# An unused strip of 192 bytes per partition, so that all large on-chip tiles begin at the same byte modulo 512

## The reference, cut to what matters

```python
scores  = scale * x @ state.T         # per batch (8) and head (8); x 512 x 64, state 32 x 64
a       = softmax(scores);   xread = a @ state
scores2 = scale * state @ x.T
a2      = softmax(scores2);  sread = a2 @ x
x = concat(xread, sread) as rows of 512          # 8 x (512 + 32) rows
h = relu(x @ w_in);  x = (h * h) @ w_out         # first block, 512 -> 2048 -> 512
out = (((x @ w1) * (x @ w2)) @ w3) @ w_out2      # second block, 512 -> 1024 -> 1024 -> 512
```

## The kernel before, in words

| stage | matmuls of 128 x 128 weights | weight from | moving from | columns |
|---|---|---|---|---|
| start, w3 x w_out2 (`multiply_w3`, L590) | 16 x 12 | v | E | 512 |
| first block, h (`h_chunk`, L617), 8 tiles | 16 x 6 a tile | G (GA, GB) | aT | 512 |
| first block, y (`y_chunk`, L625), 8 tiles | 16 x 12 a tile | X | v | 512 |
| attention scores beside it (L541 to L545) | 12 a tile | bd | x | 512 |
| attention, sread (L557 to L562) | 24 a tile | a2T | x | 256 |
| first block of the 256 state rows, h and y | 16 x 12 each | E or G; X | aT; v | 256 |
| second block, a and b (`ab_chunk`, L708), 8 tiles | 8 x 24 a tile | X | E | 512 |
| second block, out (`out_chunk`, L718), 8 tiles | 8 x 12 a tile | v | G | 512 |
| second block of the 256 state rows, a and b | 8 x 24 | X | E | 256 |
| the same, out | 8 x 6 | v | G | 512 |

## Time and profile before

### The profile page before, as it was taken

How to read it: one execution, slowest core, us unless ns; L and a number is a source line. 1 busy time by engine, 2 the same in 40 slices (tenths; PEclk the granted TensorE clock), 3 DMA queues, 4 the chain that set the end, 5 groups by cost and what they waited for, 6 DMA issues and landing times.

```text
span 1312.9 us, 15958 instructions
## 1 busy us (share of the span) xinstructions
PE 1287.8 (98%) x5977; PEld 1051.4 (80%) x5977; DVE 593.4 (45%) x974; ACT 487.0 (37%) x897; POOL 19.4 (1%) x35
## 2 busy tenths in 40 slices
PE   8979999999999999999999999999999999999996
PEld 5657888888888888888889888888888888888886
DVE  6666867565666757565546422212222222222121
ACT  6565554544544545444435321112121212111121
POOL 1000000000000000000000000000000000000000
PEclk9998999999999999999999999999999999999999
DMA  8986431121222121211214221101000100000000
GB/s 293 354 294 211 136 130 53 62 87 49 93 67 80 64 96 49 85 62 44 96 65 153 89 64 49 33 32 33 32 32 32 26 38 12 36 0 32 0 33 16
DMA packets 49815, 105.49 MB, mean 80 GB/s; under 512 B 4072, under 2 KB 5096, under 8 KB 48744
## 3 DMA queue, kind: packets, MB, share of 16 engines
q1 hardware_dynamic: 45464, 84.43, 19.4%
q0 software_dynamic: 4304, 20.45, 4.1%
HBM read 68.16 MB, written 36.70 MB: 80 GB/s over the span
## 4 chain that ended last, share of the span: by engine, by line
PE 95%; DMA 3%; DVE 1%; ACT 0%; issue 0%; SPq 0%; DVEq 0%; ACTq 0%; POOLq 0%
PE ps_y L527 47%; PE ps_h L527 30%; PE ps_t L527 17%; DMA g_scratch<-g_extra 1%; DMA wp_scratch<-stage 1%; DMA g_scratch<-stage 1%; PE ps_t L586 1%; PE ps_h L586 0%; PE ps_t L551 0%; DMA raw<-in_moe_w_in 0%; DVE v_lo L1001 0%; DVE t L1001 0%; ACT v_hi L798 0%; DVE stage L1112 0%; DVE stage L1090 0%
## 5 line engine op out<-in xcount | busy, mean ns | idle before, releaser
L1001 DVE TENSOR_TENSOR t<-t,ps_t 128x512 f32<-128x512 f32 (+1 forms) x72 | 47.4, 659 | 387.3 <-ACT t L798 387.3
L527 PE MATMUL ps_y<-v_hi,X_hi 128*128 128x512 f32 (+1 forms) x576 | 219.7, 381 | 2.1 <-DVE stage L1090 2.1
L527 PE MATMUL ps_y<-v_lo,X_hi 128*128 128x512 f32 (+1 forms) x576 | 219.2, 381 | 0.0
L527 PE MATMUL ps_y<-v_hi,X_lo 128*128 128x512 f32 (+1 forms) x576 | 219.2, 381 | 0.0
L1001 DVE TENSOR_TENSOR v_lo<-t,v_hi 128x512 fp32r<-128x512 f32 (+1 forms) x216 | 143.1, 663 | 155.2 <-ACT v_hi L798 155.2
L798 ACT CAST v_hi<-t 128x512 fp32r<-128x512 f32 (+1 forms) x216 | 128.8, 597 | 192.4 <-DVE t L1001 192.4
L798 ACT COPY t<-ps_h 128x512 f32<-128x512 f32 (+2 forms) x78 | 46.7, 598 | 398.0 <-PE ps_t L527 394.4
L884 ACT ACTIVATE t<-ps_h 128x512 f32<-128x512 f32 (+1 forms) x144 | 82.7, 574 | 166.9 <-PE ps_h L527 166.7
L1001 DVE TENSOR_TENSOR t<-t 128x512 f32<-128x512 f32 (+1 forms) x144 | 95.0, 659 | 103.4 <-ACT t L884 103.1
L527 PEld LDWEIGHTS ps_y<-v_hi,X_hi 128*128 128x128 f32 x576 | 109.0, 189 | 23.7 <-issue 2.5
L527 PEld LDWEIGHTS ps_y<-v_lo,X_hi 128*128 128x128 f32 x576 | 108.7, 189 | 21.0
(11 more groups left out here) (157 smaller groups left out, 1879.5 us busy)
## 6 DMA issues: line engine op xcount, KB each, us to landing
raw<-g_scratch SPq DMA_DIRECT2D x64, 256.0 KB
raw<-in_moe_w_in SPq DMA_DIRECT2D x32, 256.0 KB
raw<-in_x_T SPq DMA_DIRECT2D x32, 256.0 KB
raw<-in_x_tok SPq DMA_DIRECT2D x32, 256.0 KB
y_scratch<-stage POOLq DMA_DIRECT2D x8, 1024.0 KB, 5.7
raw<-y_scratch SPq DMA_DIRECT2D x32, 256.0 KB
out<-stage POOLq DMA_DIRECT2D x8, 1024.0 KB, 4.2
g_scratch<-g_extra SPq DMA_DIRECT2D x14, 512.0 KB, 6.5
```

The source lines that it names most:

```text
L527: mm = nc.tensor.matmul(dst, w, m, start=first and n == 0, stop=last and n == 2)
L1001: return nc.vector.tensor_tensor(dst, a, b, op)
```

## The change

One tile of 48 float32 (192 bytes in each partition) that nothing reads or writes is placed behind `d2`. All tiles behind it move up by 192 bytes: x_hi and E_hi begin at 160896, GA at 193664, st_hi and GB at 210048, each 128 modulo 512. No instruction is added, removed or moved; only addresses in x, s1, aT, a2T, e2, E, G, st and g_extra change.

```diff
@@ -96,6 +96,7 @@
         d1 = sb("d1", [P, HG * TB])
         m2 = sb("m2", [P, HG])
         d2 = sb("d2", [P, HG])
+        sb("line", [P, 48])
         with ExitStack() as attention:
             x_hi = sb("x_hi", [P, PAIRS, S], F32R, attention)
             with ExitStack() as softmax1:
```

## The result

The changed kernel takes 1292.69 us (median of 4 runs, 1292.21 to 1293.25) against 1314.01 for the kernel before (4 runs, 1313.48 to 1314.56): a ratio of 0.9838, 95% interval 0.9821 to 0.9855, 21.3 us. In a second set the ratio was 0.9836 (0.9822 to 0.9850), with 1292.2 us for the changed kernel (median of 4 executions, 1291.43 to 1293.46, without two disturbed ones of 1588 and 4504 us). 1291.1 us was forecast.

What follows compares the result with a forecast made beforehand. The prediction took TensorE, busy 98% of the span, as the bound: matmul count times the distance between starts. Gains of 15.4, 8.3, 0.5 and 0.2 less losses of 1.3, 0.3 and 0.2 made 22.6 us: 1291.1 us, range 1286 to 1303.

Steps and rivals of the forecast that it cites:

- Part 1: Second block, 8 tiles of 288 matmuls: 233.3 to 226.7 ns each, a gain of 15.4 us.
- part 5: 256-column products of the state rows: equal starts are slower, losing 1.3 us in a and b, 0.3 in h, 0.2 in out.
- Part 2: First block, h and y chunks: 4.15 to 4.08 us each, 9.0 us gained less 0.7 for new starts, net 8.3.
- part 3: Attention scores: six matmuls go from 1.39 to 1.36 us, a gain of 0.5 us.
- part 6: VectorE and ScalarE writes of x, E and G at new addresses: hidden by TensorE; half a microsecond either way, nothing taken.
- Part 4: The w3 product, 8 matmuls in 1.84 us: at best 0.6 us gained, 0.2 us taken.
- Addresses do nothing: Rival for the whole kernel: placement is indifferent or the strip does not arrive; time as now, 1313.7 us; chance 0.06.
- Equal starts are the slow case: Rival: 512-column matmuls with equal starts take 240 ns in long streams; 39.7 us slower, 1353.4 us; chance 0.04.
- The second block stays in its rate: Rival: second block keeps 233.3 ns even with equal starts; only 7.2 us gained, 1306.5 us; chance 0.10.
- Thrown out all the time: Rival: 512-column streams settle but keep being unsettled, averaging 229.2 ns; 10.7 us gained, 1303.0 us; chance 0.12.

Runs made afterwards that it cites:

- G alone: Against the kernel before, 192 unused bytes between E and GA: G starts at 128 modulo 512, x and E stay at 448; 1301.53 us.
- E alone: Against the kernel before, x and E moved to start at 128 modulo 512 by the 192-byte strip, G kept at 448 by 320 more; 1303.16 us.

## Why the prediction was right, step by step

**The bound and the count.** TensorE is still at 98%, with the same 5977 matmuls; no wait of another engine grew into the place of what went, but for one (below). The sum was 22.6 us; the profiled executions differ by 1314.48 - 1292.21 = 22.3, the medians by 21.3. That 22.3 is so near is in part luck: it holds 0.9 us at the start that are not the change's, about what the tiles of the first block came short (both below).

**Part 1, second block: right.** The rate of nine settled matmuls in a y chunk was the rate of 2304 in a row. Less the losses of the state rows, 13.9 us were forecast and 14.1 came. The state rows lost what part 5 priced: a and b 1.44 for 1.36, out 1.39 for 1.37, h 1.44 for 1.42.

**Part 2, first block: the mechanism right, the term too large.** With part 3 and the loss of h, 8.5 us were forecast and 7.0 came. Two terms were mis-sized. The gain per chunk, "4.15 less 4.08", was taken from rounded rows as 0.07 us (the trace's nanoseconds give 4.147 less 4.080), and the cost of each new start as 0.03. After the change y reads 2.75 behind sread as assumed, but 2.77 behind the first transposes of a tile and 2.75 to 2.76 behind the second, up to 0.05 over the settled 2.72. A tile gained 72.86 - 71.87 = 0.99 us, not the 1.1 of the sum. The scores went from 1.39 to 1.36, as part 3 has it. And in tile 0 a wait took the place of gained time, which no row of before had been asked for:

```profile
168.29 1.36 PE ps_h L528 x6
169.65 0.12 issue
169.77 3.10 PE ps_t L528 x24
```

The sread of batch 1 took 2.87 us before and takes 0.35 more now, the gap ahead of it included. The timeline of VectorE and of the weight loads after:

```profile
168.82 0.69 DVE L1002 TENSOR_TENSOR a2T_lo<-ps_t,a2T_hi 128x512 fp32r<-128x512 f32 x1
...
169.74 0.19 PEld L528 LDWEIGHTS ps_t<-x_hi,a2T_hi 128*128 128x128 f32 x1 [0.51 <-issue]
```

VectorE's last split of a2T ends at 169.51, when the h ahead of sread has 0.14 us left, and the first weight load starts at 169.74. Before, the split ended at 170.82 and sread started at 171.56, 0.74 us later. So in tile 0, with the weights still to be split beside the attention, VectorE gained 1.3 us on the clock and TensorE 1.8, and the cover of 0.74 us was used up. The profile names no releaser for the gap; it calls it issue. That it is the split is read from two more traces: in the second execution of the changed kernel and with G alone, sread starts 0.26 and 0.25 us behind the split's end, as here, and with E alone, where TensorE comes later, 0.74 us behind it and without a gap. The prediction named VectorE's idle time for part 6 only, and from other tiles.

The border between the first two rows of the table is not firm. The second execution of the changed kernel has the same two rows as follows:

```profile
L528 PE MATMUL ps_h<-aT_hi,GA x288: 283/389/501, 100.5 to 706.7; 128*128 128x512 f32 x128, 128*128 128x256 f32 x16
L528 PE MATMUL ps_h<-E_hi,X_hi x288: 277/389/396, 719.8 to 1274.5; 128*128 128x512 f32 x128, 128*128 128x256 f32 x16
```

Its first block starts 2.2 us earlier and its second only 0.8, for TensorE waits longer in tile 0 for VectorE and ScalarE (3.2 us for `stage` and 1.4 for `g_extra`, against 2.2 and 0.5). So the two rows are best taken together: 8.2 us gained, 9.0 in that execution, and 8.7 forecast. The tile distance of 0.99 us for 1.1 is the firmer sign that the term was too large.

**Part 4 and the start.** The chains before and after, at the first load and at a w3 chunk:

```profile
1.40 5.63 DMA raw<-in_moe_w_in
...
22.99 2.96 PE ps_y L527 x12
```

```profile
1.40 5.07 DMA raw<-in_moe_w_in
...
22.15 2.94 PE ps_y L528 x12
```

The w3 chunks gave 16 x 0.02 = 0.3 us for the 0.2 taken. Of the other 0.9 us, 0.56 lie in the first load, and where the first h starts differs from execution to execution: at 102.7 and at 100.5 us in two of the changed kernel. So these 0.9 us are not counted to the change. One product whose distance the strip changed stands in no part of the sum, the G products with `st` as 64-row weight; their six matmuls took 0.90 us before and 0.89 to 0.90 after, so it cost nothing to leave them out.

**Part 5: right, with the reading behind it only half right.** Equal starts cost 119 to 120 ns at 256 columns in every kernel. What was read as the price of the other distances, 113.3 or 118.3, was the price of a state. The same distance gave 113.3, 117.7 and 118 in different surroundings. The kernel before itself shows two of them, in rows that the prediction didn't look at. In the first chunk of the second block's state rows, behind an out chunk at 2.80 us, a and b take 1.41; in all later ones, behind an out chunk at 2.76 or 1.37, they take 1.36:

```profile
1263.83 2.80 PE ps_y L527 x12
1266.63 1.41 PE ps_h L527 x12
...
1269.46 2.76 PE ps_y L527 x12
1272.22 1.36 PE ps_h L527 x12
```

**The rivals.** "Addresses do nothing" fell with the result: 192 unused bytes made 2304 matmuls 6.7 ns shorter each. The Trainium skill (SBUF — State Buffer, Who interferes with whom) says that TensorE has two independent read ports and never waits on anyone. That placement is indifferent, which the prediction drew from it, is not borne out here; whether TensorE waits at a port, no run shows. "Equal starts are the slow case" is true at 256 columns only. "The second block stays in its rate" was wrong for equal starts, but what it named, more than one rate at one distance, is what the G kernel showed for unequal ones. "Thrown out all the time" fell: the chain goes from a to b to out without a change.

**What the rows did not tell.** The title's modulus. The prediction reasoned modulo 512, because every slice is a step of 512 bytes; the strip of 448 bytes showed 256. Nor is the physical reason known. Weight loads run beside the matmuls (busy 81% and 98% of the span), and in these streams the next matmul's weight starts at the same byte, modulo 256, as the matmul's own. Whether the distance to the own weight or to the next one counts was not tried.

## What to carry to other kernels

In a kernel bound by matmuls with a weight load each, compare the distance between starts (the chain's time over its count), not the duration of one, between groups of one shape. If groups differ by some per cent, look up the start addresses: here equal starts modulo 256 of weight and moving operand gave 512-column float32r streams their shortest distance, 226.7 against 229 to 233.3 ns, and a strip between tiles is all that it takes. Try other distances for narrow streams, and measure them in place, for their rate depends on what runs ahead.

## What the runs showed of the hardware that was not expected

| distance of the two groups, modulo 256 | strip | 12 of 512 columns, second block | whole kernel, us |
|---|---|---|---|
| 0 | 192 or 448 | 2.72 | 1292.7, 1292.6 |
| 32 | 224 | 2.80 | 1314.2 |
| 64 | none | 2.80 | 1314.0 |
| 128 | 64 | 2.78 to 2.79 | 1312.1 |
| 192 | 128 | 2.80 | 1310.0 |

But for the top row, each strip was timed in one execution, so the rates carry the argument and not the times. A stream of matmuls has lasting rates, and it keeps one until another shape or another distance comes between. At equal starts it is 226.7 ns (512 columns) and 120.0 (256). At unequal ones it is 233.3 ns, a cycle of 226, 229 and 232, or, at 128 bytes, a cycle of seven around 232.3; and 113.3, 117.7 or, at 32 bytes, 116.7 (1.40 us for 12) for 256 columns. With equal starts, 512-column streams came back to 226.7 ns from every entry seen, within six matmuls behind 256 columns and within ten behind transposes or behind an unequal pair. That a stage with untouched operands can change its rate for what its neighbour does, as a and b did when G alone was moved, means that part of a gain may show up in lines that the edit doesn't touch.
